# Top-k attention and routed experts on one core: votes of the last two pairs by value columns, an earlier choice of the first expert, and another order of row loads

## What is computed

```python
scores = scale * np.matmul(q, k.transpose(0, 1, 3, 2))
kth = np.partition(scores, -32, axis=-1)[..., -32:-31]
scores = np.where(scores >= kth, scores, -1e9)
attn = softmax(scores);  x = (attn @ v) as rows of 512          # 1152 tokens
logits = x @ w_gate                                             # 512 x 8
expert = argmax(logits);  gate = softmax(logits)[expert]
# per expert, up to 288 tokens in order: disp = x of its tokens
y = np.maximum(disp @ w1[e], 0) @ w2[e]                         # 512 x 1024, 1024 x 512
out[token] = gate * y[its place]                                # 0 beyond the capacity
```

## Time and profile before

| | |
|---|---|
| median of 3 runs | 455.47 us (454.4 to 455.99) |
| profiled execution | 455.4 us, its span 453.7 us |
| PE matmul | 404.4 us busy, 89% |
| DVE | 285.5 us, 63% |
| ACT | 238.0 us, 52% |
| POOL | 232.3 us, 51% |
| DMA | 57.84 MB, mean 127 GB/s |
| mean granted clock of PE | 0.987 |

### The profile page before, as it was taken

The page is one execution under the profiler, slowest core; times in us unless marked ns, Lnnn a source line. Parts: engine busy times, 40 slices in busy tenths (PEclk is TensorE's granted clock), DMA queues, the critical chain, the costliest instruction groups (busy, mean ns, idle before and its releaser), DMA issues.

```text
span 453.7 us, 8631 instructions
## 1 busy us (share of the span) xinstructions
PE 404.4 (89%) x2753; PEld 343.7 (76%) x2753; DVE 285.5 (63%) x1391; ACT 238.0 (52%) x420; POOL 232.3 (51%) x225
## 2 busy tenths in 40 slices
PE   2986778989999899897997999999899999999993
PEld 1553435777778687787787999979799999999771
DVE  2599999999999999999999964401020202122210
ACT  2233347989888889888688883132112122131320
POOL 4045467989888799899899801612001111020310
PEclk9999999999999999999799999999999999999997
DMA  4210132014060140331100106969999775777500
GB/s 104 54 42 11 30 117 53 3 38 135 2 156 19 40 135 0 93 121 72 28 2 1 28 3 230 378 219 311 372 325 315 237 258 204 255 245 234 187 22 20
DMA packets 53634, 57.84 MB, mean 127 GB/s; under 512 B 34383, under 2 KB 34383, under 8 KB 53585
## 3 DMA queue, kind: packets, MB, share of 16 engines
q1 hardware_dynamic: 51408, 52.51, 37.3%
q0 software_dynamic: 2176, 4.73, 2.8%
HBM read 45.39 MB, written 13.92 MB: 131 GB/s over the span
## 4 chain that ended last, share of the span: by engine, by line
PE 36%; POOL 5%; DMA 4%; issue 3%; ACT 2%; DVE 1%; SPq 1%; POOLq 0%; DVEq 0%; ACTq 0%
PE ps_s L869 12%; PE ps_s L887 11%; PE ps_o L669 4%; DMA scores<-dispatched 3%; PE ps_o L844 3%; PE ps_t L642 2%; POOL probs L488 2%; POOL rest L483 1%; DMA dispatched<-x,r_slot 1%; ACT pT L976 1%; PE ps_s L695 1%; PE ps_o L825 1%; POOL dispatched L497 1%; PE ps_t L813 1%; SPq L405 1%
## 5 line engine op out<-in xcount | busy, mean ns | idle before, releaser
L483 POOL TENSOR_TENSOR rest<-below,scores 128x576 f32<-128x576 f32 x69 | 96.1, 1410 | 43.8 <-DVE below L1141 43.8
L669 PE MATMUL ps_o<-v_aug,pT 128*128 128x128 f32 (+2 forms) x800 | 102.4, 278 | 0.0
L669 PEld LDWEIGHTS ps_o<-v_aug,pT 128*128 128x128 f32 (+1 forms) x800 | 95.8, 184 | 1.4 <-issue 1.4
L488 POOL TENSOR_TENSOR probs<-scores,probs 128x576 f32<-128x576 f32 x66 | 93.3, 1431 | 1.9 <-ACT probs L952 1.9
L1042 ACT ACTIVATE scores<-ps_s 128x288 f32<-128x288 f32 x64 | 26.3, 411 | 103.4 <-PE ps_s L869 103.4
L1076 DVE MAX8 cand<-scores 128x8 f32<-128x96 f32 x432 | 72.3, 240 | 12.1 <-ACT scores L926 12.1
L926 ACT ACTIVATE scores<-ps_s 128x576 f32<-128x576 f32 x72 | 46.2, 649 | 41.8 <-PE ps_s L611 24.5
L642 PE MATMUL ps_t<-ident,probs 128*128 128x128 f32 x360 | 55.6, 287 | 14.0 <-ACT pT L976 8.1
L869 PE MATMUL ps_s<-scores 128*128 128x192 f32 (+3 forms) x448 | 66.5, 306 | 0.0
L869 PEld LDWEIGHTS ps_s<-scores 128*128 128x128 f32 x448 | 64.4, 191 | 1.0 <-issue 0.7
L552 POOL DMA_INDIRECT out_dram<-yo,numbers x15 | 13.8, 917 | 100.1 <-DVE yo L1397 81.1
(11 more groups left out here) (140 smaller groups left out, 396.3 us busy)
## 6 DMA issues: line engine op xcount, KB each, us to landing
w_sb<-in_moe_w_dram SPq DMA_DIRECT2D x9, 2048.0 KB, 9.7
scores<-in_moe_w_dram SPq DMA_DIRECT2D x7, 2048.0 KB, 12.6
dispatched<-empty SPq DMA_DIRECT2D x18, 257.0 KB, 3.9
scores<-dispatched SPq DMA_DIRECT2D x21, 192.8 KB, 3.7
out_dram<-empty SPq DMA_DIRECT2D x9, 256.0 KB, 2.8
q_nat<-in_q_dram SPq DMA_DIRECT2D x16, 128.0 KB, 2.3
k_nat<-in_k_dram SPq DMA_DIRECT2D x16, 128.0 KB, 2.4
v_aug<-in_v_dram SPq DMA_DIRECT2D x16, 128.0 KB, 2.4
```

The costliest lines, as they stand in the source:

```text
L483: nc.gpsimd.tensor_tensor(rest[:, n % 3, :], below[:, n % 3, :], score_tile(n), ALU.mult).then_inc(rest_ready, 1)
L488: nc.gpsimd.tensor_tensor(probs[:, n % PROBS, 0:S], score_tile(n), probs[:, n % PROBS, 0:S], ALU.subtract).then_inc(masked_ready, 1)
L669: last = nc.tensor.matmul(dst, lhs, v_aug[:, g % 2, c, h, 0:width], start=(c == 0), stop=(c == TT - 1))
```

## The change

- The last two pairs (6 and 7) no longer go through transpose_x and logits. Instead their values v are multiplied with the 64 rows of w_gate of their head beforehand: SP loads v of both pairs once more (into columns of x that are written later) and w_gate split by head (wg_heads, cleared by DVE). At steps 16 and 20 PE transposes the values (turn_values), at 18 and 22 it multiplies them (vote); ACT copies at steps 17, 19, 21 and 23. The 16 vote columns go beside the values in v_aug (place_votes on ACT, at steps 72 and 81), so weighted_values yields each head's share of the logits in eight further columns, which DVE multiplies by the reciprocal and adds (voted).
- CHOSEN is 18 instead of 20: the router's exponential of batch 0 is on ACT two steps earlier, and the ranks of batch 0 on PE.
- assign_slots(0) stands ahead of the last three late_cuts on DVE, and choose_lead within it.
- The last head's x is written behind the choice for batch 1 (scale_head). Behind the last weighted values PE places 10 of batch 0's 20 ahead of the ranks, and nothing is transposed.
- scatter_tokens waits for the x of its own batch.
- SP loads the third expert's rows right behind the second's, ahead of the first's (which have a buffer of their own now), of w2 of the second and of w1 and w2 of the third.

The diff, without new names of buffers and semaphores:

```diff
@@ -36,15 +36,19 @@
     NEXT = 6
-    CHOSEN = 20
+    CHOSEN = 18
...
-    TURNED = {TILES * 2: 0, TILES * 3: 1, TILES * 4: 2, TILES * 5: 3, TILES * 6 - 2: 4, TILES * 6 + FULL: 5, TILES * 7 + FULL: 6}
-    SPARE = FULL * (D + 1) + P
+    TURNED = {TILES * 2: 0, TILES * 3: 1, TILES * 4: 2, TILES * 5: 3, TILES * 6 - 2: 4, TILES * 6 + FULL: 5}
+    VOTED = PAIRS - 2
+    VOTE_AT = 2 * TILES - 2
+    VOTES_AT = {TILES * (VOTED - 1) + 5: 0, TILES * VOTED + 5: 1}
+    WIDE = D + 1 + E
+    SPARE = FULL * WIDE + P
@@ -172,17 +180,19 @@
         yo = sb("yo", [P, NSUB, DM])
+        lead_rows = probs.rearrange("p u s -> p (u s)")[:, 0:NSUB * ROW].rearrange("p (j r) -> p j r", j=NSUB)
...
-        o_slots = [ps_o[:, h, 0:TT * (D + 1)].rearrange("p (t d) -> p t d", t=TT) for h in range(2)]
+        o_slots = [ps_o[:, h, 0:TT * WIDE].rearrange("p (t d) -> p t d", t=TT) for h in range(2)]
...
-        LOG += [ps_s[:, 0, 0, n * TT * E:(n + 1) * TT * E].rearrange("p (t e) -> p t e", t=TT) for n in range(CH)]
+        LOG += [ps_s[:, 0, 0, n * TT * E:(n + 1) * TT * E].rearrange("p (t e) -> p t e", t=TT) for n in range(VOTED - CH)]
+        VOTE = ps_t[:, TT * P:TT * (P + 2 * E)]
@@ -339,6 +364,12 @@
             load_qk(2)
+            sp.wait_ge(wg_clean, 1)
+            for h in range(2):
+                sp.dma_start(wg_heads[h * D:(h + 1) * D, :, h, :],
+                             w_gate.rearrange("(c h d) e -> h d c e", h=2, d=D)[h][:, CH - 2:CH]).then_inc(wg_heads_loaded, 16)
+            for i in range(2):
+                load_heads(VOTED + i, v_h, values_of(i).rearrange("p t (h d) -> p t h d", h=2), v_nat_loaded[i])
@@ -395,11 +426,8 @@
             def load_rows(k, e):
-                if k == 2:
-                    sp.wait_ge(xd_loaded[0], 16 * NSUB)
-                if k >= 2:
+                if k >= 3:
...
-                if k >= 3:
@@ -415,8 +443,8 @@
                 for part, rows in FIRST_PARTS:
-                    sp.dma_start(xd[0:rows, 0, part, :],
-                                 disp[bass.ds(e * CAP + part * P, rows), :]).then_inc(xd_loaded[0], 16)
+                    sp.dma_start(lead_rows[0:rows, part, :],
+                                 disp[bass.ds(e * CAP + part * P, rows), :]).then_inc(lead_rows_loaded, 16)
@@ -430,10 +458,14 @@
             load_rows(1, second)
+            sp.wait_ge(order_ready, 1)
+            third = expert_at(2)
+            load_rows(2, third)
...
-            sp.wait_ge(order_ready, 1)
-            for k in range(2, E):
+            load_w1(2, third)
+            load_w2(2, third)
+            for k in range(3, E):
@@ -491,7 +523,7 @@
                 pool.wait_ge(slots_ready, b + 1)
-                pool.wait_ge(pv_done, ALL)
+                pool.wait_ge(x_ready, 2 * PAIRS_PER_B * (b + 1))
@@ -577,6 +609,8 @@
             def load_and_transpose(g, transposed):
+                if g == 3:
+                    pe.wait_ge(votes_kept, 4)
@@ -650,6 +684,8 @@
                     pe.wait_ge(v_loaded[g % 2], VLOADS * (g // 2 + 1))
+                    if g >= VOTED:
+                        pe.wait_ge(votes_placed, 2 * (g - VOTED + 1))
@@ -659,12 +695,12 @@
                             r = t if t < FULL else t - FULL - 1
-                            width = D + 1 if h == 1 and r == FULL - 1 else P
-                            dst = ps_o[:, h, r * (D + 1):r * (D + 1) + width]
+                            width = WIDE if h == 1 and r == FULL - 1 else P
+                            dst = ps_o[:, h, r * WIDE:r * WIDE + width]
...
-                            dst = ps_o[0:TAIL, h, FULL * (D + 1):FULL * (D + 1) + P]
+                            dst = ps_o[0:TAIL, h, FULL * WIDE:FULL * WIDE + P]
@@ -695,6 +731,27 @@
                 last.then_inc(logits_done, 1)
+            def turn_values(i, naturals):
+                pe.wait_ge(v_nat_loaded[i], VLOADS)
+                pe.wait_ge(nat_copied, 2 * naturals)
+                if i > 0:
+                    pe.wait_ge(votes_kept, 2 * i)
+                for t in range(TT):
+                    rows = P if t < FULL else TAIL
+                    last = nc.tensor.transpose(ps_t[:, t * P:t * P + rows], values_of(i)[0:rows, t, :], ident[0:rows, 0:rows])
+                last.then_inc(vT_in_psum, 1)
+            def vote(i):
+                pe.wait_ge(vT_copied, i + 1)
+                pe.wait_ge(wg_heads_loaded, 32)
+                for t in range(TT):
+                    rows = P if t < FULL else TAIL
+                    last = nc.tensor.matmul(VOTE[0:rows, t * 2 * E:(t + 1) * 2 * E], xT[:, i, t * P:t * P + rows],
+                                            wg_heads[:, i].rearrange("p h e -> p (h e)"), start=True, stop=True)
+                last.then_inc(votes_in_psum, 1)
@@ -738,6 +795,10 @@
                     weighted_values(s - LEAD - 4)
+                if s in (VOTE_AT, VOTE_AT + 4):
+                    turn_values((s - VOTE_AT) // 4, naturals)
+                if s in (VOTE_AT + 2, VOTE_AT + 6):
+                    vote((s - VOTE_AT) // 4)
@@ -761,14 +822,11 @@
             pe.wait_ge(hot_placed, TT)
-            place_first_batch(0, 4)
-            transpose_x(2 * CH - 1, ALL)
-            place_first_batch(4, 7)
-            logits(2 * CH - 1)
+            place_first_batch(0, 10)
...
-            place_first_batch(7, 13)
...
-            place_first_batch(13, CH * TT)
+            place_first_batch(10, CH * TT)
+            pe.wait_ge(x_ready, 2 * PAIRS)
@@ -788,14 +846,14 @@
-                pe.wait_ge(xd_loaded[0], 16 * NSUB)
+                pe.wait_ge(lead_rows_loaded, 16 * NSUB)
...
-                                                   xd[0:rows, 0, part, c * P:(c + 1) * P], ident[0:rows, 0:rows])
+                                                   lead_rows[0:rows, part, c * P:(c + 1) * P], ident[0:rows, 0:rows])
@@ -981,6 +1039,25 @@
+            def copy_vT(i):
+                act.wait_ge(vT_in_psum, i + 1)
+                nc.scalar.activation(xT[:, i, 0:S], ps_t[:, 0:S], ACT.Copy).then_inc(vT_copied, 1)
+            def keep_votes(i):
+                act.wait_ge(votes_in_psum, i + 1)
+                nc.scalar.activation(votes[:, i, 0:FULL], VOTE[:, 0:FULL * 2 * E].rearrange("p (t h e) -> p t h e", t=FULL, h=2),
+                                     ACT.Copy).then_inc(votes_kept, 1)
+                nc.scalar.activation(votes[0:TAIL, i, FULL], VOTE[0:TAIL, FULL * 2 * E:].rearrange("p (h e) -> p h e", h=2),
+                                     ACT.Copy).then_inc(votes_kept, 1)
+            def place_votes(i):
+                g = VOTED + i
+                act.wait_ge(votes_kept, 4)
+                act.wait_ge(pv_done, TILES * (g - 1))
+                nc.scalar.activation(v_aug[:, g % 2, 0:FULL, :, D + 1:WIDE], votes[:, i, 0:FULL], ACT.Copy).then_inc(votes_placed, 1)
+                nc.scalar.activation(v_aug[0:TAIL, g % 2, FULL, :, D + 1:WIDE], votes[0:TAIL, i, FULL],
+                                     ACT.Copy).then_inc(votes_placed, 1)
@@ -999,6 +1076,12 @@
                         copy_pair(s // TILES + 1)
+                if s in (VOTE_AT + 1, VOTE_AT + 5):
+                    copy_vT((s - VOTE_AT) // 4)
+                if s in (VOTE_AT + 3, VOTE_AT + 7):
+                    keep_votes((s - VOTE_AT) // 4)
+                if p in VOTES_AT:
+                    place_votes(VOTES_AT[p])
@@ -1007,7 +1090,6 @@
                     router_exponentials(0)
-            copy_xT(2 * CH - 1)
@@ -1212,6 +1293,17 @@
                     add_logits(g - 2)
+                if g >= VOTED:
+                    nc.vector.tensor_tensor(voted[:, n - 2 * VOTED], o_slots[h][:, :, D + 1:WIDE],
+                                            rden[:, h, :].unsqueeze(2).to_broadcast([P, TT, E]),
+                                            ALU.mult).then_inc(voted_ready, 1)
+                if n < 2 * PAIRS - 1:
+                    scale_head(n)
+            def scale_head(n):
+                g, h = divmod(n, 2)
+                col = (g // PAIRS_PER_B) * PITCH + (g % PAIRS_PER_B) * 2 * D + h * D
@@ -1228,9 +1320,11 @@
             def choose_experts(b):
-                if b == B - 1:
-                    add_logits(PAIRS - 1)
-                dve.wait_ge(log_read, CH * (b + 1))
+                if b == 0:
+                    dve.wait_ge(log_read, CH)
+                else:
+                    dve.wait_ge(voted_ready, 4)
+                    link(nc.vector.tensor_tensor(r_log[:, b], r_log[:, b], voted[:, 3], ALU.add))
@@ -1251,6 +1345,7 @@
                                                         op0=ALU.mult, op1=ALU.add))
+                    choose_lead()
@@ -1318,6 +1413,7 @@
             nc.vector.memset(ps_t[:, :], 0.0).then_inc(psum_clean, 1)
+            nc.vector.memset(wg_heads[:, :, :, :], 0.0).then_inc(wg_clean, 1)
@@ -1360,21 +1456,27 @@
             recheck(CHECKS - 1, count_bad(CHECKS - 1))
+            assign_slots(0)
...
-            assign_slots(0)
-            choose_lead()
...
```

(15 more changed lines are left out.)

20 lines of the change are left out of this document (18 added, 2 removed).

## The result

The changed kernel takes **452.78 us** (median of 10 executions, 450.78 to 453.85), the kernel before 455.29 in the same comparison (10 executions). The ratio is 0.9934, 95% interval 0.9910 to 0.9958. A second comparison (c1_again, 12 executions) gave 452.30 us against 454.62 and 0.9952, 0.9927 to 0.9977. The ratios here are the recorded estimates over the single executions; the quotients of the two medians are 0.9945 and 0.9949, gains of 2.5 and 2.3 us. The profiled execution took 453.23 us, span 451.5; that of c1_again had span 451.0.

The account below looks back on a forecast made before the run. DVE was taken to bound the kernel up to about 210 us and PE from about 240 us on. Terms +2.0 + 0.2 - 1.2 - 1.9 - 2.15 = -3.05 us took 455.47 to 452.4 us, range 449.9 to 455.0.

Parts of the forecast that it names:

- early loss: Value transposes at step 16 delay step 17's scores, so DVE waits before tile 13: +2.0 us, bounds +1.6 and +3.1.
- from there to the last threshold: ACT's small vote-column copies at about 223 and 243 us, beside POOL's masks: +0.2 us, bounds 0 and +0.4.
- Part 2: End of attention: PE loses pair 6's transposes and logits, ACT's router exponential moves earlier: gain 1.2 us, bounds 0.5 and 1.9.
- Part 3: Last weighted values to first expert: 10.0 us of PE placing instead of 11.9, gain 1.9, bounds 1.5 and 2.0.
- first to second expert: Stretch from first to second expert's start, where the forecast expected no new wait for the second's rows: 0 us.
- Part 4: Third expert's rows requested earlier, so PE's 2.19 us gap before them goes: gain 2.15 us, bounds 2.2 and 0.
- margin at tile 13: Near 53 us, DVE's tile 13 needs the 18th score copy; slack put at under 0.1 us.
- in full: Rival: PE stays slow, the second pair's pick is 3.1 us late and ACT's copies cost 0.4: 453.7 us, chance 0.15.
- side way: Near 77 to 80 us, POOL's mask waits for ACT and DVE for its pick; DVE could be about 3.1 us late.
- toll: CHOSEN = 18 makes ACT wait for r_dif before its router exponential; PE's next transposes come 0.75 us later.
- no new wait, with 1 us to spare: Second expert's rows follow the scatter, whose slots come 3.1 us earlier; PE wants the rows only 1.9 us earlier.
- a w2 slowed by its successors: Rival: second expert's w2 shares bandwidth with later loads and lands 4.2 us too late: 456.6 us, chance 0.07.

Follow-up runs that it names:

- c1_again: The changed kernel unedited, run again for a second profile and more times: 452.30 us, ratio 0.9952 to the kernel before.
- e4: Changed kernel with batch 0's scatter held back until all weighted values are done: 450.53 us, ratio 0.9920 to the kernel before.
- e3: Changed kernel with the third expert's rows issued behind w2 of the second again: 453.17 us, ratio 0.9955 to the kernel before.
- e5: Changed kernel with the five value transposes of step 16 made twice: 453.69 us, ratio 0.9978 to the kernel before.
- e2: Changed kernel with CHOSEN back at 20 and assign_slots(0) behind the last three late cuts: 455.03 us, ratio 1.0003 to the kernel before.
- e6: Changed kernel with the second expert's w1 requested behind that expert's rows: median 455.62 us, ratio 0.9998 to the kernel before.
- e1: Changed kernel with the first turn at step 17 and first vote at 19, not 16 and 18: 450.22 us, ratio 0.9918.

## Why the prediction was right, and where it wasn't

Predicted 452.4 us, measured 452.78. The sum against the span was -3.05, measured -2.2 (after) and -2.7 (c1_again); the medians give -2.5 and -2.3. The forecast was counted from 455.47, and the kernel before took 455.29 in the comparison, so 0.2 us of the close hit is the base. Its terms:

| term | predicted | after | c1_again |
|---|---|---|---|
| early loss, to 212 us | +2.0 | +1.99 | +2.46 |
| from there to the last threshold | +0.2 | +0.91 | +0.02 |
| last threshold to last values (Part 2) | -1.2 | -0.54 | -1.31 |
| last values to first expert (Part 3) | -1.9 | -2.01 | -2.54 |
| first to second expert | 0 | -0.11 | +1.10 |
| second expert's gap (Part 4) | -2.15 | -2.35 | -2.35 |

- **Early loss.** Place, releaser and size were right: 2.15 us of waiting, 1.99 at 212 us. Of c1_again's 2.46 a good 0.3 stood before the turn; from the k transposes on both profiles lose 2.1. That the margin at tile 13 was under 0.1 us was right as well. What I had missed is the spread, and it has two sources. I took the level to be slow at 50 us and asked only when it rises behind 60: it is up at 49 in five of the profiles (with the turn once at step 16 the wait for scores is none to 0.9 us there, and the loss 0.7 to 0.9, in e4 all of it from the checks), and not before 79 in e3, where DVE waited 1.52 us for the pick and the loss is 3.0 (166.5 - 163.5), near the rival "in full". And I left out DVE's waits for the row of checks, 0.5 us before and up to 3.4 in e5. The side way exists as told: DVE's wait for the pick was 0.42 us before, 0.59 after, 1.52 in e3.
- **place_votes** shows no cost (c1_again +0.02). The +0.91 of the first profile doesn't come back in it: in the first profile DVE waited up to 1.5 us for the landing of the row of checks. These are the rows of its waits from 225 to 262 us (us in total, times, longest), of before, after and c1_again:

```profile
DVE worst L1163 <- DMA bad_row<-bad: 0.7, 1, 0.7
```

```profile
DVE worst L1245 <- DMA bad_row<-bad: 2.2, 2, 1.5
```

```profile
DVE worst L1245 <- DMA bad_row<-bad: 0.9, 1, 0.9
```

- **Part 2.** -1.31 where ScalarE's late copy didn't fall in, 1.2 predicted. ScalarE's idle before the router exponential was 0.76 us (0.9 predicted), PE's next transposes 0.56 us late (0.75 predicted). The late cuts were covered. But the prediction treated the early choice as a toll alone; without it (e2) the kernel is slower, by PE's wait for the second expert's rows and the lower clock behind it, so it buys more than the toll.
- **Part 3.** The size was too small: 9.3 us from the last values' reciprocal to the end of the last placing in c1_again (282.26 to 291.60), 10.0 predicted: the first placings start 0.26 us ahead of the reciprocal, and carry and ranks take 0.4 us of PE (284.28 to 284.66), 0.6 predicted. **The step that failed is "no new wait, with 1 us to spare"** for the second expert's rows. The scatter's last issue came 3.1 us earlier as predicted: it ended 12.3 us behind the last values' reciprocal in c1_again, 15.5 before. What I had put at nothing is a longer landing: from the end of that issue to the request of the rows it took 4.6 us before, 5.3 and 6.0 after. I let the rows follow the slots; they follow the end of a stretch in which three 2 MB loads and both scatters fill the DMA engines, and this stretch starts with the lead weights, only 1.85 us earlier than before (273.16 against 275.01). They were requested at 301.12, before at 301.15. PE stood 0.99 us before them in c1_again; in the first profile ScalarE's delay of about that size hid it. e6 shows the cause: 2 MB less, and the landing takes 2.2 us.
- **Part 4** was right in the traces: gap gone, w2 of the second expert no wait (issued at 307.99, used at 319.69). It was tight: in c1_again it was issued at 307.49, landed after 11.1 us at 318.6 and was used at 319.18. e3 brings 2.41 us back in its profile, though not in its median. One reading behind this part was wrong. The 11.9 us of the earlier trace rows is the median of the two loads at 275.01 and 275.51; they landed after 8.0 and 15.9. So the second was slowed more than I read and the first no more, which still speaks against a w2 slowed by its successors.

No run puts the transposes and logits of the last two pairs back alone, so the gains of Parts 2 and 3 are read from the timelines and not isolated.

The total came out right partly by luck. In c1_again a loss that was missed (1.1) and a larger early loss (0.5) were met by gains that were undersized (0.6 in Part 3, 0.2 in Part 4, 0.1 in Part 2) and by a cost that didn't come (0.2); in the first profile the sum misses by 0.9 us, mostly through the waits for the checks and ScalarE's late copy. The early loss alone differs between profiles of kernels with the turn once at step 16 by 2.3 us (0.7 to 3.0), while the changed kernel's times spread over 3.1 (450.8 to 453.9).

The fastest kernel measured is e1, 450.22 us. Its lead over the changed kernel (0.9918 against 0.9934 and 0.9952) lies within the intervals; that the early wait is gone is shown with step 17's scores at either pace, but not with the slow pace lasting longer.

## What to carry to other kernels

Where a fixed order puts new work ahead of an operation with no margin, put it one step behind: here one place in the list decides over 2 us where PE runs at the slow pace. Before calling a later transfer covered, ask which stretch of full DMA engines it stands behind and when that stretch starts; moving 2 MB out of it moved a small load by 3.8 us, and moved the wait to the 2 MB. Two edits that are each good may not add: measure the pair. And where an edit costs time, check that the wait stands where the edit acts: in e5 the expected size came from two waits elsewhere.
